# Thresholds of the top-score mask computed on ScalarE for each lane, and the output scaling placed between the two score passes

## The reference, cut to what matters

```python
def _attn_ref(q, k, v, tau):
    scores = scale * np.matmul(q, k.transpose(0, 1, 3, 2))
    thresh = np.max(scores, axis=-1, keepdims=True) - tau
    scores = np.where(scores >= thresh, scores, -1000000000.0)
    scores = scores - np.max(scores, axis=-1, keepdims=True)
    attn = np.exp(scores)
    attn = attn / (np.sum(attn, axis=-1, keepdims=True) + 1e-09)
    return np.matmul(attn, v).astype(np.float32)

def reference(**kwargs):
    attn_out = _attn_ref(...)
    x = attn_out.transpose(0, 2, 1, 3).reshape(B * S, H * D)
    x = _moe_ref(x=x, ...)
    return _moe2_ref(x=x, ...)
```

## Time and profile before

| | |
|---|---|
| median of three runs | 1045.88 us (1045.74 to 1046.98) |
| the profiled execution | 1045.74 us, of which the span of the trace is 1044.1 us |
| PE busy over the span | 1013.5 us, 97% |
| DVE busy | 634.3 us, 61% |
| ACT busy | 503.1 us, 48% |
| POOL busy | 556.7 us, 53% |

### The profile page before, as it was taken

The page is one execution under the profiler, slowest core; times in us unless marked ns, Lnnn a source line. Parts: engine busy times, 40 slices in busy tenths (PEclk is TensorE's granted clock), DMA queues, the critical chain, the costliest instruction groups (busy, mean ns, idle before and its releaser), DMA issues.

```text
span 1044.1 us, 21287 instructions
## 1 busy us (share of the span) xinstructions
PE 1013.5 (97%) x6920; PEld 858.9 (82%) x6920; DVE 634.3 (61%) x1556; ACT 503.1 (48%) x1020; POOL 556.7 (53%) x576
## 2 busy tenths in 40 slices
PE   9999999999958999999999999999999999999996
PEld 6778888787627888888888889999999999999995
DVE  7999999999763222222222228667666666666663
ACT  5777777777562222222222225455555545455542
POOL 2344343421427778985720727866556565565564
PEclk9999999999978999999999999999999999999999
DMA  9176544642437899997824646110000000000000
GB/s 251 40 216 190 164 130 137 170 123 81 152 101 212 287 285 348 360 323 220 273 88 181 185 145 197 42 31 31 31 1 31 31 20 28 13 30 0 11 21 30
DMA packets 101126, 135.95 MB, mean 130 GB/s; under 512 B 34800, under 2 KB 52464, under 8 KB 100528
## 3 DMA queue, kind: packets, MB, share of 16 engines
q1 hardware_dynamic: 72688, 66.54, 21.7%
q0 software_dynamic: 22336, 60.30, 18.5%
q10 hardware_dynamic: 6016, 7.96, 2.2%
HBM read 118.78 MB, written 16.00 MB: 129 GB/s over the span
## 4 chain that ended last, share of the span: by engine, by line
PE 93%; DVE 3%; issue 2%; ACT 1%; DMA 0%; POOLq 0%; POOL 0%; DVEq 0%; ACTq 0%
PE ps L1196 22%; PE ps L1198 22%; PE ps L1197 22%; PE ps L1091 7%; PE ps L1034 4%; PE ps L1062 3%; PE ps L1056 3%; PE ps L1222 2%; PE ps L1043 2%; PE ps L1101 1%; PE ps L1083 1%; DVE sc L1402 1%; PE ps L1192 1%; PE ps L1019 1%; PE ps L1134 1%
## 5 line engine op out<-in xcount | busy, mean ns | idle before, releaser
L652 POOL TENSOR_TENSOR wl<-stage,wh 128x512 fp32r<-128x512 f32 x128 | 161.7, 1291 | 31.7 <-DMA stage<-w 15.3
L771 POOL TENSOR_TENSOR mg<-mw,mr 128x384 f32<-128x384 f32 x96 | 117.4, 1223 | 73.9 <-DVE mr L1638 73.5
L829 ACT ACTIVATE ex<-sc,rmin 128x576 f32<-128x576 f32 x144 | 108.9, 776 | 68.8 <-DVE sc L1402 68.8
L777 POOL TENSOR_TENSOR gl<-mg,gh 128x384 fp32r<-128x384 f32 x96 | 98.1, 1022 | 79.2 <-ACT gh L967 78.3
L1196 PE MATMUL ps<-yth,winh 128*128 128x384 f32 x384 | 131.0, 341 | 0.0
L1198 PE MATMUL ps<-yth,winl 128*128 128x384 f32 x384 | 129.5, 337 | 0.0
L1197 PE MATMUL ps<-ytl,winh 128*128 128x384 f32 x384 | 128.9, 336 | 0.0
L1402 DVE TENSOR_SCALAR_CACHE_REDUCE sc<-ps,nscale 128x576 f32<-128x576 f32 x144 | 112.0, 815 | 7.3 <-PE ps L1043 3.8
L1197 PE MATMUL ps<-woutl,gh 128*128 128x512 f32 x288 | 113.5, 394 | 0.0
L1196 PE MATMUL ps<-wouth,gh 128*128 128x512 f32 x288 | 113.0, 392 | 0.0
L1198 PE MATMUL ps<-wouth,gl 128*128 128x512 f32 x288 | 112.0, 389 | 0.0
(11 more groups left out here) (205 smaller groups left out, 2410.2 us busy)
## 6 DMA issues: line engine op xcount, KB each, us to landing
stage<-w SPq DMA_DIRECT2D x128, 256.0 KB, 5.6
wh<-w POOLq DMA_DIRECT2D x32, 1024.0 KB, 8.1
y_dense<-yo ACTq DMA_DIRECT2D x25, 256.5 KB, 4.9
k_t<-kT SPq DMA_DIRECT2D x16, 288.0 KB, 4.3
vb<-v SPq DMA_DIRECT2D x16, 288.0 KB, 4.6
q_t<-qT SPq DMA_DIRECT2D x15, 288.0 KB, 3.6
stage<-w_in SPq DMA_DIRECT2D x16, 256.0 KB, 3.2
winh<-w_in POOLq DMA_DIRECT2D x1, 4096.0 KB, 13.9
```

What stands on the lines that cost most here:

```text
L652: g.tensor_tensor(dst, raw, src.bitcast(F32), ALU.subtract).then_inc(w_split, 1)
L771: g.tensor_tensor(mg[:, f % 2, :], mw[:, f % 2, :], mr[:, f % 2, :], ALU.mult).then_inc(g_done, 1)
L777: g.tensor_tensor(gl[:, f % 4, :], mg[:, f % 2, :], gh[:, f % 4, :].bitcast(F32), ALU.subtract).then_inc(gl_ready, 1)
L829: act.activation(ex[:, i % 2, t * S:(t + 1) * S], sc[:, i % 2, t * S:(t + 1) * S], ACT.Exp, bias=rmin[:, i % 2, t:t + 1], scale=-1.0).then ...
```

## The change

`thresholds` on DVE, one instruction of 128x2 for each unit, is removed. ACT computes each lane's threshold in an instruction of its own, 128x1, ahead of that lane's exponential; `thr_ready` now counts lanes instead of units. On DVE `norm(i)` moves from behind both score passes to a place between them, and the explicit wait for `out_done` ahead of the second pass goes, since `norm` has the same wait. PE's wait for `normed` ahead of `scores` is removed.

```diff
@@ exp(body, i), ACT
+                act.activation(thr[:, i % 2, t:t + 1], rmin[:, i % 2, t:t + 1], ACT.Identity,
+                               bias=taup[:, :]).then_inc(thr_ready, 1)
                 act.activation(ex[...], sc[...], ACT.Exp,
                                bias=rmin[:, i % 2, t:t + 1], scale=-1.0).then_inc(exp_done, 1)
@@ scores(body, i), PE
             wait(pe, max_done, tiles_before(body, i))
-            wait(pe, normed, unit(body, i) - 3)
@@ DVE
-        def thresholds(body, i):
-            dve.wait_ge(max_done, tiles_before(body, i) + LANES)
-            dve.tensor_scalar(thr[:, i % 2, :], rmin[:, i % 2, :], taup[:, :], None, ALU.add).then_inc(thr_ready, 1)
-
@@ mask(body, i, t), DVE
-            dve.wait_ge(thr_ready, unit(body, i) + 1)
+            dve.wait_ge(thr_ready, n + 1)
@@ attention(b, last), DVE
+                norm(b, i)
                 if ahead:
-                    dve.wait_ge(out_done, unit(b, i) + 1)
                     copy_max(b, i + 3, 1)
-                    thresholds(b, i + 3)
-                norm(b, i)
@@ the first three units, DVE
-            thresholds(0, i)
```

## The result

The changed kernel takes 1050.62 us (median of five runs, 1050.35 to 1052.61), the kernel before 1045.74 us (five runs): a ratio of 1.0053, 95% interval 1.0043 to 1.0064. That is 4.9 us slower; the forecast was +4.9, with slower as the likeliest direction. Further executions of the changed kernel are on record, thirty in all; they spread from 1050.28 to 1053.73 us with a median of 1051.1, so the agreement to a tenth is luck. The profiled execution is the longest of them, 1053.7 us.

A forecast was written before the change was run, and what follows sets the result against it. PE was taken to set the pace in ordinary units, DVE just under it. Ordinary units 2.7 plus tails 2.5 less 0.3 for the stall gave +4.9 us on 1045.74, that is 1050.6 us; range 1044.5 to 1054.0.

The forecast's parts named there:

- the ordinary units: Split-score units away from tails: late `pt` copy costs PE 0.13 us every two units, 2.7 us over 42 units.
- the tails: Units scaling a tail's output: scaling ahead of the second pass delays PE 0.36 us net, seven times, 2.5 us.
- the stall: One DVE threshold held to 1.16 us beside a POOL instruction: moving it returns 0 to 0.5 us, taken as 0.3.
- DVE's relief: Threshold removed from DVE: 0.25 us a unit less, hidden by PE in ordinary units, so worth 0.
- The step on ACT: Time from a new 128x1 threshold on ACT to its next instruction: 0.21 us, bounds 0.05 and 0.30.
- The first threshold free, the second exponential 0.41 late: ACT in ordinary units: first threshold delays nothing; `norm` (0.20) and second threshold (0.21) delay the second exponential 0.41 us.
- Unsplit bodies: Two attention bodies with costlier fp32 scores: the ring there has slack, so no loss counted, T to T still 3.80.
- Removing PE's wait: PE's wait for `normed` ahead of scores: already implied by `max_done` in ordinary units, so removal is worth 0.
- the sign to look for: If right, PE idles before its L1062 transposes, put down to ACT's L840, where it had no idle time.
- No difference: Rival: ACT step nearer 0.05 or more PE slack before the transposes; within 0.2%, about 1046.8 us; chance 0.21.
- Faster: Rival: copies have room, so relief at tails and from the stall remains, -2.9 us, 1042.8; chance 0.12.
- The ring through DVE: Rival: DVE's ring, 0.03 us to spare, closes through ACT, adding in every unit; 1053 to 1055 us; chance 0.08.

The follow-up runs named there:

- no_thr_behind: Kernel before with no threshold instruction, the mask comparing exponentials with a constant, `norm` behind both passes: 1042.95 us, 0.9970 of the kernel before.
- twice_first: Changed kernel plus one more 128x1 ACT instruction a unit ahead of the first exponential, its new tile shifting others by 32 bytes: 1061.09 us.
- merged_copy: Changed kernel with the last two `pt` copies as one of 640 columns: 1049.64 us, 1.0041 of the kernel before.
- after_pe_wait: Changed kernel with PE's wait for `normed` put back: 1053.12 us, 1.0057 of the kernel before.
- norm_between: Kernel before with only `norm` moved between the score passes, thresholds still on DVE: 1049.14 us, 1.0019 of the kernel before.
- act_thr: Kernel before with only the thresholds moved to ACT; `norm` and PE's wait stay: 1047.67 us, 1.0005 of the kernel before.
- pad32: Changed kernel with an unused tile of 32 bytes a partition, no instruction added: 1058.49 us, 1.0122 of the kernel before.
- twice_second: Changed kernel plus one more 128x1 ACT instruction a unit ahead of the second exponential, its new tile shifting others by 32 bytes: 1065.56 us.
- pad64: Changed kernel with an unused tile of 64 bytes a partition, no instruction added: 1051.27 us, 1.0051 of the kernel before.
- again_second: Changed kernel plus one more 128x1 ACT instruction ahead of the second exponential, with a 64-byte tile: 1057.29 us, 1.0114 of the kernel before.

## Why the prediction was right, point by point

The mechanism was right: the last `pt` copy comes late and PE, through it, every second T. The sum was closer than its terms. In attention the ordinary units cost about 2.1 where 2.7 was forecast, the tails 2.9 where 2.5 was, and the stall gave back about 0.5 where 0.3 was; 4.46 against 4.9. The last 0.4 came from behind attention, where nothing had been forecast, so that the totals meet at +4.9 is luck.

- **PE sets the pace, DVE's relief is worth 0 in ordinary units.** Right: DVE's busy time fell by 1.6 in 50 us and no ordinary T of a split or unsplit body came sooner away from the stall. no_thr_behind shows what the relief is worth, 1.9 us at tails and 0.8 in the body of the stall.
- **The step on ACT, 0.21.** Measured 0.20 (209.22 to 209.42). The working had a slip: 0.31/384 is 0.81 ns a column and not 0.83, which would have made the step 0.23 and the sum a few tenths higher. The Trainium skill (ScalarE: Activation LUTs, What ACT_TABLE_LOAD costs) leads to 0.19; the trace has a duration of 0.29 us for it and a step of 0.20, so both fit within 0.01. Its table sets hold too: the changed kernel's trace has one table load, as before.
- **The first threshold free, the second exponential 0.41 late.** Measured T + 1.99 for T + 2.01. The first exponential's step ended at about 208.49 + 0.69 = 209.18, before the second threshold's 209.22, so the first threshold was indeed free. twice_first shows that this place has hardly more room: one more instruction there cost 1.96 us.
- **0.13 for every two ordinary units.** Measured 3.61 + 3.75 = 7.36 in the pair shown against twice 3.62, 0.12; 0.11 in most. Besides, a split body loses it three times and not the three and a half of 42 units, together 2.1 for 2.7. merged_copy moves this term: the later of two distances falls from 3.73 to 3.67.
- **Tails 0.36 each.** Measured scores 0.40 later after T, and about 0.41 in the four distances at a tail, 2.9 for 2.5. Part of the late transposes came from the output copy, which the forecast didn't have late there.
- **Unsplit bodies 0.** Right for the ordinary units there.
- **The stall, 0.3 back.** Some 0.5 measured, and the stall did not go: the mask took the threshold's place, which the forecast had left open. The Trainium skill's rule on the shared port pair (SBUF — State Buffer, SBUF: two separate sides) had said so; the row agrees (1.45 us beside a POOL instruction). But my reading of it, that nothing comes back, didn't hold: T to T fell from 4.41 to 3.98. Why isn't shown. It isn't PE's wait: with the wait back (after_pe_wait) it is 3.98 too, and in norm_between, where the scaling stands ahead of a threshold held to 1.01 us, it is 4.37. What fits is how long DVE was held: 0.93 us before and 4.41, 0.78 in norm_between and 4.37, 0.64 in the changed kernel and 3.98, and in no_thr_behind, where a mask took 1.11 us, 0.30 and 3.62, no loss at all.
- **Removing PE's wait, 0.** Right: 258.90 and 258.89.
- **Where I misjudged the sign to look for.** I expected PE's idle time to be put down to the pt copy. The table of waits, 50 to 290 us, names the output copy:

```profile
PEld ps L1102 <- ACT ot L848: 15.3, 46, 0.9
...
PE ps L1102 <- ACT ot L848: 5.6, 10, 0.8
```

Of the 46, 26 are the 0.16 or 0.17 us that PE's weight loads show in this place before the change too, when nearly all were put down to "issue". Only starts in the timeline tell which copy PE really waits for, and merged_copy settles it for the pt copy in ordinary units. At tails both are late: PE is idle 0.59 for the output copy, and after the four transposes that follow it waits again, until 0.15 after the end of the `pt` copy.
- **The rivals.** "No difference" fell with the step at 0.20. "Faster" fell at the tails above all: the second exponential came 1.1 us later after T there (2.71 for about 1.6), more than the copies had room for, and the transposes came 0.57 late. The ring through DVE had room as worked out (0.03), since every second T still came after 3.61 or 3.62, and it closed when a second instruction was added. No table was loaded for the threshold.

## What to carry to other kernels

When the engine that sets the pace waits for nothing, an instruction taken off the second-busiest engine is worth nothing, and the question is what the receiving engine has queued behind the new one. Write down, from starts in a timeline, how much room each handover to the pacing engine has: two moves that cost little alone (+0.3 and +1.8) can cost more than double together. A total near zero need not be nothing either: in act_thr 0.6 us lost in five bodies were hidden by a stall that shrank in another. And put an experiment's extra tile where it shifts no other tile, or test the shift by itself.

## What the runs showed of the hardware

- With the tiles of the `x` region 32 bytes a partition further on and the weights where they were, the matmuls behind attention were up to 1.5% slower (389 to 395 ns for those on `wl`), 7 to 9 us in all (pad32, twice_second, twice_first); with everything 64 bytes further on they weren't (pad64, again_second).
- A DVE instruction that reads two SBUF tiles (a mask) was held by a POOL elementwise instruction: 1.45 us for 0.81, one of 144 masks. It was also the only mask of the changed kernel's trace that met such an instruction for more than 0.15 us. Score passes, which read PSUM, lay wholly beside one in places and kept their 0.82 (for example at 253.31).
- A 128x1 instruction on ACT with a bias from a tile took 0.29 us and stepped 0.20; PE started 0.15 us after the end of the ACT copy that it waited for.
